# A tuned attention and two-layer MoE kernel: attention scores by 32-query chunks with their own 64 keys, instead of 128-row products with a mask

## Chip, cores and metric

The kernel runs on one core of a Trainium2 chip, in float32. The metric is the device time of one execution in microseconds, here the median of three runs: 516.09 us (515.79 to 516.44).

## What is computed

Attention over 2 batches x 8 heads x 768 positions with head dimension 64. Queries are taken in chunks of 32. A chunk sees 16 keys to its left, its own 32, 8 to its right, and 8 memory keys: 64 keys in all, fewer at the ends of a sequence.

```python
for c in range(S // 32):
    l_start, r_end = max(0, c * 32 - 16), min(S, c * 32 + 32 + 8)
    k_full = np.concatenate([mem_k, k[:, :, l_start:r_end]], axis=2)
    v_full = np.concatenate([mem_v, v[:, :, l_start:r_end]], axis=2)
    scores = scale * np.matmul(q_c, k_full.transpose(0, 1, 3, 2))
    a = np.exp(scores - np.max(scores, axis=-1, keepdims=True))
    a = a / (np.sum(a, axis=-1, keepdims=True) + 1e-09)
    out[:, :, chunk] = np.matmul(a, v_full)
```

The result (1536 tokens x 512) goes through a dense layer pair, `h = x @ w_in; g = h * sigmoid(1.702 h); y = g @ w_out` (512 to 2048 to 512), and then through a mixture of 8 experts with one expert per token (512 to 1024 to 512), of which each takes at most 384 tokens. All this behind the attention is the same in both kernels.

## The kernel before

**Tiles.** The 1536 tokens are 12 tiles (`NT`) of 128. In a tile there are two windows of 64 queries (`WINDOWS`, `HALF`) and four pairs of heads (`NP`): `NBL` = 8 blocks. A block is one pair of heads in one window. Its 128 rows are 64 queries of the first head and 64 of the second; its columns are `KEYS` = 96 keys: 64 + 16 + 8 and 8 memory keys. The two heads of a pair share one product over 128 contraction rows, 64 per head. For this `fill_block` copies the loaded queries (`queries`) into a block-diagonal arrangement in `tile_in`, whose other places `zero_blocks` cleared at the start. The copies are ScalarE's (two per tile), and for the first three tiles one of the two is VectorE's.

**Steps of a tile t.** `scores(t)` on TensorE: 8 products of 128 x 96 into two PSUM banks. `add_mask(t)` on VectorE adds the mask (keys outside a row's chunk get -1e30) and reduces the maximum over 96 keys. `less_max(t)` on GpSimd subtracts it, `exps(t)` on ScalarE takes the exponential, `inverse(t)` on VectorE sums and inverts, `normalise(t)` on GpSimd multiplies, `transposes(t)` on TensorE turns the 8 blocks, `copy_pT(t)` on ScalarE brings them to SBUF, `values(t)` on TensorE multiplies by the values (16 products of 64 columns, alternately for the upper and lower 64 partitions of the result), and `x_high(t)` (ScalarE) and `x_low(t)` (VectorE) split the result into two parts for the dense layer. A float32 product shows as two instructions in the profile.

**Order.** Every engine has a list written out by hand, and semaphores tie them. TensorE: `keep_warm` products on a constant, scores of tiles 0 to 2, more `keep_warm`, then for each t `transposes(t)`, `scores(t + 3)`, `values(t)`. With t = 8 the values move one place later; from t = 10 on `dense_hidden` takes the place of the scores. VectorE splits the first weight units (`split_lo`) in places 9 to 11, after ScalarE's `split_hi`.

**Loads.** All loads are issued by SyncE in program order: queries, keys and values of a tile as three transfers (256, 336 and 384 KB), a ring of three tiles (`NSLOT`), which waits for the copies, the scores and the values of the tile three before. The mask (288 KB) stands between the first and the second tile's loads. The weight units (512 KB) begin with t = 11 (`EARLY_FROM`).

Of the kernel before, what the change touches and what calls it, by code (L numbers as in the profile page):

```python
# [12 lines left out]
F32 = mybir.dt.float32  # L13
# [11 lines left out]
def build(nc, dims, attn_in, mask_in, w_units, w_gate_in, gate_rows_in, const_in, out):  # L25
# [11 lines left out]
    NBL = NP * WINDOWS  # L37
    BPG = NBL // 2
    GROUPS = [(g, g + BPG) for g in range(0, NBL, BPG)]
    NG = len(GROUPS)  # L40

    MAX_GROUPS = [GROUPS] + [[(0, NBL)]] * (B * S // P - 1)
    max_done = lambda t, g: sum(len(x) for x in MAX_GROUPS[:t]) + g + 1
    SCALE = 1.0 / D ** 0.5
    QK = NBL * P + NP * SPAN
    ATT = QK + WINDOWS * DM
    Q_IN = NBL * HALF
    NSLOT = 3
# [12 lines left out]
    EARLY_FROM = NT - 1  # L61
# [13 lines left out]
    WARM_FIRST, WARM_SECOND = 34, 35  # L75
# [15 lines left out]
    with ctx:  # L91
# [40 lines left out]
        queries = []  # L132
        for i in range(NSLOT):
            queries.append(at(f"queries{i}", [P, Q_IN], F32, o))
            o += Q_IN * 4
        prob, masked = [], []
        for i in range(2):
            prob.append(at(f"prob{i}", [P, NBL, KEYS + 1], F32, o))
            o += NBL * (KEYS + 1) * 4
        for i in range(2):  # L140
            masked.append(at(f"masked{i}", [P, NBL, KEYS], F32, o))
            o += NBL * KEYS * 4
        mask = at("mask", [P, 3, WINDOWS * KEYS], F32, o)
        o += 3 * WINDOWS * KEYS * 4
# [85 lines left out]
        score_bank, pT_bank, xT_bank = (bank[0:2], [bank[2], bank[5]]), bank[3:5], bank[6:8]  # L230
# [17 lines left out]
        s_block = [sem(f"s_block{i}") for i in range(2)]  # L248
        s_tiny = sem("s_tiny")
        s_v = [sem(f"s_v{i}") for i in range(NSLOT)]  # L250
        s_zero_q = sem("s_zero_q")
        s_mask_in = sem("s_mask_in")
# [6 lines left out]
        s_mask = sem("s_mask")  # L259
# [78 lines left out]
        def query_block(n, half, place):  # L338

            return tile_in[n][half * D:(half + 1) * D, 0:NBL * P].rearrange("p (x m) -> p x m", x=NBL)[
                :, :, place * HALF:(place + 1) * HALF]

        def fill_block(write, engine, t, half):
            n = t % NSLOT
            engine.wait_ge(s_q[n], 16 * (t // NSLOT + 1))
            if t >= NSLOT:
                engine.wait_ge(s_score, NG * (t - NSLOT + 1))
            there = queries[n][half * D:(half + 1) * D, :].rearrange("p (x m) -> p x m", x=NBL)  # L350
            write(query_block(n, half, half), there).then_inc(s_block[half], 1)
# [72 lines left out]
        def _(sp):  # L424
            def load_queries(t):
                n = t % NSLOT
                if t >= NSLOT:
                    for half in range(2):
                        sp.wait_ge(s_block[half], t - NSLOT + 1)
                sp.dma_start(queries[n][:, :], attn_in[t, :, 0:Q_IN]).then_inc(s_q[n], 16)  # L430

            def load_keys(t):
                n = t % NSLOT
                if t >= NSLOT:
                    sp.wait_ge(s_score, NG * (t - NSLOT + 1))
                sp.dma_start(tile_in[n][:, NBL * P:QK], attn_in[t, :, Q_IN:Q_IN + NP * SPAN]).then_inc(s_k[n], 16)

            def load_values(t):
                n = t % NSLOT
                if t >= NSLOT:  # L440
                    sp.wait_ge(s_pv, t - NSLOT + 1)
                there = attn_in[t, 0:KEYS, Q_IN + NP * SPAN:Q_IN + NP * SPAN + WINDOWS * DM]
                sp.dma_start(tile_in[n][0:KEYS, QK:ATT], there).then_inc(s_v[n], 16)
# [30 lines left out]
            for t in range(NSLOT, NT + NSLOT):  # L474
                if t < NT:
                    load_queries(t)
                    load_keys(t)
                if t == EARLY_FROM:
                    load_unit(unit)
                    unit += 1  # L480
                if t - NSLOT + 1 < NT:
                    load_values(t - NSLOT + 1)
                if t > EARLY_FROM:
                    load_unit(unit)
                    unit += 1
# [31 lines left out]
        def _(pool):  # L517
            pool.memset(empty_row[:, 0:DM + 1], 0.0).then_inc(s_empty, 1)
            pool.memset(empty_row[:, DM + 1:ROW], FAR).then_inc(s_empty, 1)
            pool.memset(ident[:, :], 0.0).then_inc(s_pool_c, 1)  # L520
            pool.memset(ones[:, :], 1.0).then_inc(s_pool_c, 1)
# [5 lines left out]

            def by_row(stats, x0, x1):
                return stats[:, x0:x1].rearrange("p (x a) -> p x a", a=1).to_broadcast([P, x1 - x0, KEYS])

            def less_max(t):
                for g, (x0, x1) in enumerate(GROUPS):
                    for n, some in enumerate(MAX_GROUPS[t]):
                        if some[0] == x0:
                            pool.wait_ge(s_max, max_done(t, n))
                    part = masked[t % 2][:, x0:x1, :]
# [1241 lines left out]
```

## Time and profile before

| what | value |
|---|---|
| median of 3 runs | 516.09 us |
| profiled execution | 516.33 us, span of the core 514.6 us |
| instructions | 8465 |
| busy share PE / PE weight load / DVE / ACT / POOL | 97 / 81 / 64 / 46 / 36% |
| TensorE clock granted (mean) | 0.995 of full speed |
| transfers | 77.17 MB, mean 150 GB/s |
| attention part | from the start to about 63 us, where the first output of the dense layer starts |

PE is TensorE's matmuls, PEld its weight loads, DVE VectorE, ACT ScalarE, POOL GpSimd, SPq the transfers issued from SyncE's queue. The busy shares are means over the whole span; the attention part is one eighth of it, and it has other limits than the rest. "L1271" is line 1271 of the kernel: L1271 are the scores, L1282 the transposes, L1298 the values, L1470 the warm-up products, L1306 to L1308 `dense_hidden`, L1350 to L1352 the dense outputs, L885 the mask add, L869 the maximum, L537 `less_max`, L543 `normalise`, L622 the exponential, L655 and L351 the query copies, L904 `x_low`, L430, L436 and L443 the issues of queries, keys and values, L373 `split_lo`.

### The profile page before, as it was taken

To read this page: it belongs to the slowest core of one execution; us is meant where nothing else is said; L and a number is where in the kernel's file an instruction comes from. 1 tells how busy PE (TensorE), PEld (TensorE's weight loads), DVE (VectorE), ACT (ScalarE), POOL (GpSimd) and SP (SyncE) were. 2 spreads that over 40 slices of the span, in tenths; PEclk is the share of its full clock that TensorE was granted. 3 is DMA by queue.
4 is the path that set the end of the run, shared out by engine and by line. 5 is a ranking of instruction groups with operands and counts; after the bars stand their busy time and mean duration, and the time that the engine had idled before them with its cause. 6 is when DMAs were issued, how large, how long until landed. Compare 5 with 4: busy or idle time off the path is not lost.

```text
span 514.6 us, 8465 instructions
## 1 busy us (share of the span) xinstructions
PE 497.4 (97%) x3013; PEld 418.7 (81%) x3013; DVE 327.1 (64%) x688; ACT 235.6 (46%) x416; POOL 186.3 (36%) x210
## 2 busy tenths in 40 slices
PE   7999999999999999999999999999999999999993
PEld 7898788888888887888888778888988888888882
DVE  7899765445237777323776877864577878638750
ACT  3899653343231122123122365523467768847620
POOL 3887400000000000300000017245337999999942
PEclk9999999999999999999999999999999999999998
DMA  8997799700020000100222236223796987956100
GB/s 260 257 265 235 279 357 332 249 3 0 2 82 2 0 1 0 58 26 36 88 82 83 82 101 227 82 75 107 234 343 212 351 329 263 356 211 230 39 28 33
DMA packets 28588, 77.17 MB, mean 150 GB/s; under 512 B 5487, under 2 KB 5487, under 8 KB 28272
## 3 DMA queue, kind: packets, MB, share of 16 engines
q1 hardware_dynamic: 24528, 70.07, 41.0%
q0 software_dynamic: 4000, 6.32, 3.4%
q8 instruction: 35, 0.57, 0.5%
q14 instruction: 25, 0.20, 0.1%
HBM read 63.21 MB, written 19.96 MB: 162 GB/s over the span
## 4 chain that ended last, share of the span: by engine, by line
PE 83%; DVE 6%; issue 4%; ACT 2%; POOL 1%; DMA 1%; DVEq 1%; SPq 0%; another core or an unknown queue 0%; ACTq 0%; POOLq 0%
PE bank L1306 9%; PE bank L1308 9%; PE bank L1307 9%; PE bank L1350 8%; PE bank L1351 8%; PE bank L1352 8%; PE bank L1319 7%; PE bank L1271 3%; PE bank L1577 3%; PE bank L1321 3%; PE bank L1579 2%; PE bank L1580 2%; PE bank L1581 2%; PE bank L1298 2%; PE bank L1282 2%
## 5 line engine op out<-in xcount | busy, mean ns | idle before, releaser
L557 POOL DMA_INDIRECT dispatched_rows<-rows,slot_idx x12 | 13.1, 1092 | 260.5 <-issue 157.6
L373 POOL TENSOR_TENSOR w_lo<-raw,w_hi 128x256 fp32r<-128x256 f32 x100 | 88.9, 923 | 9.5 <-ACT w_hi L357 9.5
L644 ACT ACTIVATE g<-bank 128x512 f32<-128x512 f32 x48 | 28.7, 598 | 126.9 <-PE bank L1308 126.8
L357 ACT ACTIVATE w_hi<-raw 128x1024 fp32r<-128x1024 f32 x80 | 82.0, 1050 | 0.1
L373 DVE TENSOR_TENSOR w_lo<-raw,w_hi 128x1024 fp32r<-128x1024 f32 (+1 forms) x61 | 72.0, 1190 | 8.8 <-ACT w_hi L357 7.7
L911 DVE SCALAR_TENSOR_TENSOR g<-g,bank 128x512 f32<-128x512 f32 x48 | 33.0, 687 | 69.1 <-ACT g L644 69.0
L1306 PE MATMUL bank<-x_hi,w_hi 128*128 128x512 f32 x192 | 76.1, 397 | 0.0
L1350 PE MATMUL bank<-w_hi,g_hi 128*128 128x512 f32 x192 | 76.0, 396 | 0.0
L1351 PE MATMUL bank<-w_lo,g_hi 128*128 128x512 f32 x192 | 75.8, 395 | 0.0
L1352 PE MATMUL bank<-w_hi,g_lo 128*128 128x512 f32 x192 | 75.8, 395 | 0.0
L1308 PE MATMUL bank<-x_hi,w_lo 128*128 128x512 f32 x192 | 75.6, 394 | 0.0
L1307 PE MATMUL bank<-x_lo,w_hi 128*128 128x512 f32 x192 | 75.4, 393 | 0.0
L1319 PE MATMUL bank<-e_in,w_hi 128*128 128x384 f32 (+1 forms) x224 | 61.4, 355 | 1.6 <-DVE gx_lo L1173 0.9
L916 DVE TENSOR_TENSOR g_lo<-g,g_hi 128x512 fp32r<-128x512 f32 x48 | 33.2, 693 | 32.8 <-ACT g_hi L651 32.1
L1321 PE MATMUL bank<-e_in,w_lo 128*128 128x192 f32 (+1 forms) x224 | 53.6, 239 | 0.0
L651 ACT ACTIVATE g_hi<-g 128x512 fp32r<-128x512 f32 x48 | 30.4, 632 | 41.9 <-DVE g L911 40.3
L1319 PEld LDWEIGHTS bank<-e_in,w_hi 128*128 128x128 f32 x224 | 42.0, 188 | 5.5 <-issue 2.0
L972 DVE SCALAR_TENSOR_TENSOR products<-rows,gate_rows 128x512 f32<-128x512 f32 x64 | 44.2, 690 | 1.7
L1350 PEld LDWEIGHTS bank<-w_hi,g_hi 128*128 128x128 f32 x192 | 36.1, 188 | 8.7 <-DVE g_lo L916 0.2
L1352 PEld LDWEIGHTS bank<-w_hi,g_lo 128*128 128x128 f32 x192 | 36.1, 188 | 8.6
L1308 PEld LDWEIGHTS bank<-x_hi,w_lo 128*128 128x128 f32 x192 | 36.0, 188 | 8.5
L1351 PEld LDWEIGHTS bank<-w_lo,g_hi 128*128 128x128 f32 x192 | 36.1, 188 | 8.5
(155 smaller groups left out, 904.1 us busy)
## 6 DMA issues: line engine op xcount, KB each, us to landing
raw<-expert_units SPq DMA_DIRECT2D x64, 512.0 KB, 6.6
raw<-dense_units SPq DMA_DIRECT2D x16, 512.0 KB, 6.5
dispatched_rows<-empty SPq DMA_DIRECT2D x26, 257.0 KB, 11.0
slot_rows<-dispatched_rows SPq DMA_DIRECT2D x26, 257.0 KB
tile_in<-attention_tiles SPq DMA_DIRECT2D x12, 384.0 KB, 4.5
tile_in<-attention_tiles SPq DMA_DIRECT2D x12, 336.0 KB, 5.6
queries<-attention_tiles SPq DMA_DIRECT2D x12, 256.0 KB, 4.8
gate_rows<-gate_rows SPq DMA_DIRECT2D x2, 1024.0 KB, 5.0
```

Of the source, the lines that this page charges most:

```text
L357: act.activation(w_hi[u % RING][:, :], raw[u % RING][:, :], ACT.Copy).then_inc(s_whi, 1)
L373: last = engine.tensor_tensor(w_lo[u % RING][:, part], raw[u % RING][:, part], w_hi[u % RING][:, part].bitcast(F32), ALU.subtract)
L916: dve.tensor_tensor(g_lo[i % 2][:, :], g32[i % 2][:, :], g_hi[i % 2][:, :].bitcast(F32), ALU.subtract).then_inc(s_glo, 1)
L972: link(dve.scalar_tensor_tensor(products[:, :], rows[:, j, 0:DM], 1.0, gate_rows[e // HALF_E][:, e % HALF_E, :], ALU.mult, ALU.mult, accum ...
L1306: pe.matmul(dst, hi[w_at], m_hi, start=first, stop=False)
L1307: pe.matmul(dst, hi[w_at], m_lo, start=False, stop=False)
L1308: return pe.matmul(dst, lo[w_at], m_hi, start=False, stop=last)
L1319: pe.matmul(both, w_hi[u % RING][:, c:c + P], parts[:, :, k, 0:cols], start=(k == 0), stop=False)
L1321: last = pe.matmul(h[:, 0:cols], w_lo[u % RING][:, c:c + P], x_high[:, k, 0:cols], start=False, stop=(k == KT - 1))
L1350: pe.matmul(banks[j][:, :], gh, hi[:, cols], start=(f == 0), stop=False)
L1351: pe.matmul(banks[j][:, :], gh, lo[:, cols], start=False, stop=False)
L1352: last = pe.matmul(banks[j][:, :], gl, hi[:, cols], start=False, stop=(f == nf - 1))
```

## The change

A block is now one chunk of 32 queries of four heads (`QUAD`): 8 blocks (`NBL`) of 4 x 32 = 128 rows, each with the 64 keys of its chunk (`OWN`). A block's scores are four products, one per head: 64 contraction rows (the head's half of the partitions), 32 query columns, 64 keys, each written to its own 32 partitions. The host places the memory keys so that a chunk's 64 keys are adjacent. Nothing has to be zero around the queries, so they are loaded straight into `tile_in`, and query copies, zeroing and the mask go. At the two ends of a sequence `edges` writes -1e30 over the keys that don't exist (4 of the 12 tiles). `less_max` is VectorE's and reads PSUM. The weights are still written 96 wide, with zeros where a chunk has no key (set once), so that transposes and values keep their sizes. The ring has four tiles, and the keys are issued by ScalarE. All eight blocks of a tile lie in one PSUM bank, and the transposed weights get four banks. Warm-up products: 32 and 24 instead of 34 and 35. The loads of gate weights and constants move to t = 7.

```diff
+    OWN = LEFT + CHUNK + RIGHT + M
+    QUAD = P // CHUNK
+    CPW = HALF // CHUNK
+    NBL = H // QUAD * (P // CHUNK)
+    BPG = NBL // WINDOWS
-    NSLOT = 3
+    PLACE = KEYS + 1
+    NSLOT = 4
+    LEAD = 3
-    WARM_FIRST, WARM_SECOND = 34, 35
+    WARM_FIRST, WARM_SECOND = 32, 24
...
+        def part_scores(t, x0, x1):
+            side = xT_bank[0] if PARTS[t][0][1] < NBL and x0 else score_bank[t % 2]
+            return side[:, x0 * OWN:x1 * OWN].rearrange("p (x k) -> p x k", k=OWN)
...
+        def load_keys(act, t):
+            n = t % NSLOT
+            if t >= NSLOT:
+                act.wait_ge(s_score, NG * (t - NSLOT + 1))
+            act.dma_start(tile_in[n][:, Q_IN:QK], attn_in[t, :, Q_IN:QK]).then_inc(s_k[n], 16)
...
# SyncE
-            for t in range(NSLOT):
+            for t in range(LEAD):
                 load_queries(t)
-                load_keys(t)
-                if t == 0:
-                    sp.dma_start(mask[:, :, :], mask_in).then_inc(s_mask_in, 16)
             load_values(0)
-            sp.dma_start(w_gate[:, :, :], w_gate_in).then_inc(s_const_in, 16)
-            sp.dma_start(const[:, :], const_in).then_inc(s_const_in, 16)
...
# GpSimd
+            pool.memset(ones[:, :], 1.0).then_inc(s_pool_c, 1)
             pool.memset(ident[:, :], 0.0).then_inc(s_pool_c, 1)
...
-            less_max(0)
             for t in range(NT):
-                if t + 1 < NT - 1:
-                    less_max(t + 1)
                 normalise(t)
...
# ScalarE
             for t in range(NSLOT):
-                blocks(t)
+                load_keys(act, t)
             for t in range(-2, NT + 1):
+                if 1 <= t <= NT and t != NT - 3:
+                    x_high(t - 1)
                 if 0 <= t < NT:
                     copy_pT(t)
-                if 1 <= t <= NT:
+                if t == NT - 3:
                     x_high(t - 1)
                 if t + 2 < NT:
                     exps(t + 2)
-                    if NSLOT <= t + 4 < NT:
-                        blocks(t + 4)
+                    if t + 2 + NSLOT < NT:
+                        load_keys(act, t + 2 + NSLOT)
...
# VectorE
+            def maximum(t, n):
+                x0, x1 = PARTS[t][n]
+                if n == 0:
+                    edges(t)
+                dve.wait_ge(s_score, NG * t + (NG if x1 == NBL else 1))
+                dve.tensor_reduce(neg_max[t % 2][:, x0:x1], part_scores(t, x0, x1), AX.X, ALU.max,
                                   negate=True).then_inc(s_max, 1)
+            def less_max(t, n):
+                x0, x1 = PARTS[t][n]
                 if t >= 2:
+                    dve.wait_ge(s_exp, parts_done(t - 2))
+                dve.wait_ge(s_max, parts_done(t, n))
+                dve.tensor_tensor(less[t % 2][:, x0:x1, :], part_scores(t, x0, x1), by_row(neg_max[t % 2], x0, x1),
+                                  ALU.add).then_inc(s_sub, 1)
...
+            for n in range(NG):
+                maximum(0, n)
+                less_max(0, n)
+            maximum(1, 0)
+            inverse(0)
+            less_max(1, 0)
+            maximum(2, 0)
+            less_max(2, 0)
+            for t in range(NT + 1):
+                if t + 1 < NT - 1:
                     inverse(t + 1)
                 if t == NT - 1:
                     gated(0)
+                if t >= 1:
                     x_low(t - 1)
+                if t + LEAD < NT:
+                    maximum(t + LEAD, 0)
+                    less_max(t + LEAD, 0)
                 if t == NT - 3:
+                    split_lo(dve, 0)
                     inverse(NT - 1)
...
# TensorE
+                for x0, x1 in GROUPS:
+                    dst = part_scores(t, x0, x1)
                     for x in range(x0, x1):
-                        q0, k0 = x * P, NBL * P + x // WINDOWS * SPAN + x % WINDOWS * (HALF + M)
-                        last = pe.matmul(score_bank[t % 2][g][:, (x - x0) * KEYS:(x - x0 + 1) * KEYS],
-                                         tile_in[n][:, q0:q0 + P], tile_in[n][:, k0:k0 + KEYS],
-                                         start=True, stop=True)
+                        w, g, c = x // BPG, x % BPG // CPW, x % CPW
+                        for j in range(QUAD):
+                            pair, side = (QUAD * g + j) // 2, slice(j % 2 * D, (j % 2 + 1) * D)
+                            q0 = pair * P + w * HALF + c * CHUNK
+                            k0 = Q_IN + pair * SPAN + w * (HALF + M) + c * CHUNK
+                            last = pe.matmul(dst[j * CHUNK:(j + 1) * CHUNK, x - x0, :], tile_in[n][side, q0:q0 + CHUNK],
+                                             tile_in[n][side, k0:k0 + OWN], start=True, stop=True)
...
-            pe.wait_ge(s_pool_c, 2)
+            pe.wait_ge(s_pool_c, 1)
             keep_warm(WARM_FIRST)
-            for t in range(NSLOT):
-                pe.wait_ge(s_zero_q, 2 * (t + 1))
+            for t in range(LEAD):
                 scores(t)
```

## Rows read from the trace of the kernel before

**Rows 1.** The page: busy time of each engine, share of the span, instructions.

```profile
PE 497.4 (97%) x3013; PEld 418.7 (81%) x3013; DVE 327.1 (64%) x688; ACT 235.6 (46%) x416; POOL 186.3 (36%) x210
```

**Rows 2.** Stretches: length, busy time of each engine, PE clock, DMA share, GB/s.

```profile
2.50:18.00 15.50, 13.40 (x140) 12.64 (x139) 11.76 (x25) 7.22 (x13) 7.61 (x10) 1.00 1.03 288
...
15.80:48.70 32.90, 32.90 (x468) 31.47 (x465) 29.49 (x50) 30.78 (x60) 27.40 (x35) 1.00 0.90 259
```

**Rows 3.** The chain of waits up to 70 us: start, duration, what.

```profile
2.18 4.85 DMA queries<-attention_tiles
...
19.00 1.01 PE bank L1282 x8
...
43.12 1.76 PE bank L1271 x16
44.88 1.08 PE bank L1298 x32
45.96 1.01 PE bank L1282 x8
46.97 1.77 PE bank L1271 x16
...
51.11 2.60 POOL prob L543 x2
...
54.40 0.23 PE bank L1306
...
63.29 0.43 PE bank L1350
```

**Rows 4.** The timeline of the attention part: start, duration, engine, line, operation.

```profile
1.24 0.42 SPq L436 DMA_DIRECT2D tile_in<-attention_tiles  x1
...
1.70 3.34 PE L1470 MATMUL bank<-ones 128*128 128x128 bf16 x34 [1.70 <-POOL ones L521]
...
4.88 1.98 PE L1271 MATMUL bank<-tile_in 128*128 128x96 f32 x16
...
7.95 2.00 PE L1271 MATMUL bank<-tile_in 128*128 128x96 f32 x16 [1.10 <-DMA tile_in<-attention_tiles]
...
12.25 2.12 PE L1470 MATMUL bank<-ones 128*128 128x128 bf16 x35
...
14.82 1.33 PE L1282 MATMUL bank<-ident,prob 128*96 128x128 f32 x8 [0.46 <-POOL prob L543]
...
51.76 1.25 DVE L373 TENSOR_TENSOR w_lo<-raw,w_hi 128x1024 fp32r<-128x1024 f32 x1
```

**Rows 5.** Values products (L1298) in flight, stretches of 10 ns; count in brackets.

```profile
25.54:25.55 0.01, 0.00 (x1) 1.00 0.78 205
25.55:25.56 0.01, 0.01 (x2) 1.00 0.00 0
...
25.66:25.67 0.01, 0.01 (x4) 1.00 1.31 410
...
25.72:25.73 0.01, 0.01 (x6) 1.00 2.33 614
```

**Rows 6.** Groups by shape from 0 to 62 us: busy us, mean ns, idle before.

```profile
L543 POOL TENSOR_TENSOR prob<-prob,prob_inv 128x384 f32<-128x384 f32 x24 | 20.3, 868 | 3.8 <-DVE prob_inv L899 3.1
...
L655 ACT ACTIVATE tile_in<-queries 64x512 f32<-64x512 f32 x21 | 13.1, 623 | 5.6 <-DMA queries<-attention_tiles 5.4
L885 DVE TENSOR_TENSOR masked<-bank,mask 128x384 f32<-128x384 f32 x24 | 12.8, 545 | 2.9 <-PE bank L1271 2.6 <-issue 0.3
...
L622 ACT ACTIVATE prob<-masked 128x384 f32<-128x384 f32 x24 | 11.6, 518 | 6.0 <-POOL masked L537 5.7
...
L869 DVE TENSOR_REDUCE neg_max<-masked 128x8 f32<-128x768 f32 x11 | 10.4, 948 | 0.3
L904 DVE TENSOR_TENSOR x_lo<-bank,x_hi 128x512 fp32r<-128x512 f32 x11 | 7.5, 682 | 0.4 <-ACT x_hi L636 0.4
...
L869 DVE TENSOR_REDUCE neg_max<-masked 128x4 f32<-128x384 f32 x2 | 1.1, 553 | 0.1
```

More of the change, by code:

```diff
@@ L131, in build @@
             o += ATT * 4
[L132 to L136, printed above, removed]
+        prob, less = [], []
         for i in range(2):
-            prob.append(at(f"prob{i}", [P, NBL, KEYS + 1], F32, o))
-            o += NBL * (KEYS + 1) * 4
+            prob.append(at(f"prob{i}", [P, NBL, PLACE], F32, o))
+            o += NBL * PLACE * 4
         for i in range(2):
[L141 to L144, printed above, removed]
+            less.append(at(f"less{i}", [P, NBL, OWN], F32, o))
+            o += NBL * OWN * 4
         probT = []
@@ L427, in load_queries @@
                 if t >= NSLOT:
[L428 to L434, printed above, removed]
                     sp.wait_ge(s_score, NG * (t - NSLOT + 1))
-                sp.dma_start(tile_in[n][:, NBL * P:QK], attn_in[t, :, Q_IN:Q_IN + NP * SPAN]).then_inc(s_k[n], 16)
+                sp.dma_start(tile_in[n][:, 0:Q_IN], attn_in[t, :, 0:Q_IN]).then_inc(s_q[n], 16)
             def load_values(t):
@@ L651, in g_high @@
                 act.activation(g_hi[i % 2][:, :], g32[i % 2][:, :], ACT.Copy).then_inc(s_ghi, 1)
-            def blocks(t):
-                for half in range(1 if t < NSLOT else 2):
-                    fill_block(lambda to, there: act.activation(to, there, ACT.Copy), act, t, half)
             for t in range(NSLOT):
-                blocks(t)
+                load_keys(act, t)
             for t in range(-2, NT + 1):
+                if 1 <= t <= NT and t != NT - 3:
+                    x_high(t - 1)
                 if 0 <= t < NT:
                     copy_pT(t)
-                if 1 <= t <= NT:
+                if t == NT - 3:
                     x_high(t - 1)
@@ new lines, in edges @@
+            def edges(t):
+                place = t % TPB
+                if place == 0:
+                    ends = part_scores(t, 0, BPG)[:, 0:BPG:CPW, 0:LEFT]
+                elif place == TPB - 1:
+                    ends = part_scores(t, NBL - BPG, NBL)[:, CPW - 1:BPG:CPW, OWN - RIGHT:OWN]
+                else:
+                    return
+                dve.wait_ge(s_score, NG * t + (1 if t == 0 else NG))
+                dve.memset(ends, -1e30).then_inc(s_edge, 1)
+                dve.wait_ge(s_edge, sum(x % TPB in (0, TPB - 1) for x in range(t + 1)))
@@ L1704 @@
     f32 = np.float32
+    memory_at = [w * (half + M) + 2 * CHUNK - M for w in range(2)]
+    key = np.arange(P + LEFT + RIGHT)
+    place_of = key + M * (key >= memory_at[0]) + M * (key >= memory_at[1] - M)
     attn = np.zeros((NT, P, q_in + H // 2 * span + 2 * DM), f32)
@@ L1716 @@
         for wide, own, memory in ((kw, k, mem_k), (vw, v, mem_v)):
-            wide[:, M + lo - s0 + LEFT:M + hi - s0 + LEFT] = own[b, :, lo:hi]
-            wide[:, 0:M] = memory[b]
-            wide[:, span - M:] = memory[b]
+            wide[:, place_of[lo - s0 + LEFT:hi - s0 + LEFT]] = own[b, :, lo:hi]
+            for at in memory_at:
+                wide[:, at:at + M] = memory[b]
         attn[t, :, q_in:q_in + H // 2 * span] = kw.reshape(H // 2, 2, span, D).transpose(1, 3, 0, 2).reshape(P, -1)
@@ L1723 @@
             attn[t, 0:keys, at:at + DM] = vw[:, w * (half + M):w * (half + M) + keys].transpose(1, 0, 2).reshape(keys, DM)
-    mask = np.full((P, 3, 2, keys), -1e30, f32)
-    for r in range(P):
-        u0 = r % half // CHUNK * CHUNK
-        for w in range(2):
-            at = M * (1 - w) + u0
-            mask[r, :, w, at:at + LEFT + CHUNK + RIGHT] = 0.0
-    mask[:, 0, 0, M:M + LEFT] = -1e30
-    mask[:, 2, 1, keys - M - RIGHT:keys - M] = -1e30
-    mask[:, :, 0, 0:M] = 0.0
-    mask[:, :, 1, keys - M:] = 0.0
-    mask = mask.reshape(P, 3, 2 * keys)
     def in_units(w):
@@ L1764 @@
     nc = bacc.Bacc("TRN2", target_bir_lowering=False, num_devices=1)
-    arrays = {"attention_tiles": attn, "masks": mask, "dense_units": dense, "expert_units": experts,
+    arrays = {"attention_tiles": attn, "dense_units": dense, "expert_units": experts,
               "gate_weights": gate_w, "gate_rows": gate_rows, "constants": const}
```

192 lines of the change are left out of this document (73 added, 119 removed).

## The prediction

> **What bounds the kernel now.** I read the page's engine line first: the span is 514.6 us and PE is busy for 97% of it [rows 1]. That says only that PE seldom waits, so I asked next for the stretches. Between 15.8 and 48.7 us, nearly the whole attention part that the change touches, PE is busy all the time, ACT 94%, DVE 90%, POOL 83%, and the DMA engines move 259 GB/s at a share of 0.90 [rows 2]. Four engines and the DMA are within 17% of the same limit, so a part taken from DVE, ACT or POOL gives nothing by itself. The chain of waits decides: from 19.0 to 48.7 us it holds PE alone, in a pattern of three groups per tile, transposes 1.01, scores 1.76, values 1.08 [rows 3]. The sum, 3.85 us, is the pitch; the pattern stands eight times. At the ends other engines enter the chain. At the start the second tile's queries land at 7.03 us [rows 3], and the first transposes start at 14.82 [rows 4]. At the end POOL's normalisation takes 2.60 us of the chain, the first dense product starts at 54.40 and the first dense output at 63.29 [rows 3]. After that nothing is touched, so I count until there: what the change saves at 63.29 it saves in the whole.
>
> **Scores on PE, the deciding term.** Now a tile has 8 products of 128 x 96, two instructions each: 16 in 1.76 us, 110 ns apiece [rows 3]. After the change it has 8 x 4 = 32 products, with half the contraction (64), 32 columns of stationary operand and 64 moving columns: 64 instructions. No such shape is in the trace. Nearest is the values product: also 64 moving columns, stationary 64 wide, its results going alternately to the two halves of the partitions. Its starts come two at a time: the count of those in flight goes 1, 2, then 4 at 25.66 and 6 at 25.72 [rows 5], and 32 take 1.08 us [rows 3]. So after a first gap of 110 ns a pair costs about 59 ns, an instruction 29.5 ns. Three readings fit: fp32 operands stream at about half speed (53 ns for 64 columns at 2.4 GHz), two column groups at a time; or the two passes run one after the other at full speed (26.7 ns each); or the 64-column load is the limit. The transposes, 8 in 1.01 us with 128 moving columns and only 96 loaded, against 110 ns for 128 loaded in the scores [rows 3], speak for a streaming limit. Under the first two readings 64 moving columns cost what they cost in values: 64 x 29.5 = 1.89 us. The shape of the array changes once more per tile (the transposes and the scores now use the same one, later they don't), for which I take the 0.11 us of the first gap in values. Sum 2.00 us, so 0.24 us more per tile than now, and a pitch of 1.01 + 2.00 + 1.08 = 4.09 us. Bounds: below, the third reading, a load half as wide, 32 pairs of 29 to 32 ns, 1.0 + 0.11 = 1.1 us; above, no overlap at all, 64 x 59 = 3.8 + 0.11 = 3.9 us. I take 2.00, the row with the same moving width.
>
> The Trainium skill (TensorE: Matmul & The Clock Gate, "Wait — 56ns, not 53.3ns?") gives a floor of about 25 ns between starts of matmuls; the pairs that start within 10 ns [rows 5] don't obey it, but as a mean rate it would make 64 x 25 = 1.6 us, between my value and the lower bound.
>
> **DVE, ACT, POOL.** DVE loses the mask add (2 x 545 ns) and gets the subtraction of the maximum from POOL. That is 512 elements now, as long as x_lo from PSUM, 682 ns. The reductions shrink from 768 to 512 elements: between 553 (384) and 948 (768) that is 685 ns, twice [rows 6]. Per tile 0.68 + 0.68 + 0.69 + 0.20 (the reciprocal) + 0.68 = 2.9 us where it is 3.9. ACT loses the query copies (2 x 623), its exponential becomes one of about 0.6 us (now 2 x 518 [rows 6]), and it gets one issue of keys, at most the 0.42 us that it takes on SyncE's queue [rows 4]; behind that issue stand the next tile's copies, which have the slack: 2.7 us of 4.09. POOL keeps the normalisation with 256 instead of 384 elements, about 0.57 instead of 0.87 each [rows 6], 1.1 us. All this lies beside PE's 4.09 and costs nothing; if PE's groups came to 1.1 us, DMA and not these would be next.
>
> **DMA.** The bytes per tile stay: 262 + 344 + 393 KB = 1.00 MB. Gone are the 0.29 MB of masks, and the gate weights and constants go behind. While the queue is saturated, from 2.5 to 18 us, it moves 288 GB/s [rows 2]: 3.47 us per tile, under 4.09, so the transfers are hidden, but nothing below 3.47 can be had.
>
> **The start, step by step.** Warm-up products start at 1.70 now [rows 4] because `ones` is the fourth memset; it becomes the first, and they end near 4.3. The first queries and keys (0.61 MB) land at about 4.8, so the first scores run 4.8 to 6.8; the copies and zeroing are no longer before them, but the start (4.88 now [rows 4]) stays. For the second tile 1.21 MB must have come. Now 1.16 MB are ahead of the queries' landing at 7.03 [rows 3] (mask included), so scores(1) runs from 7.2 (now 7.95) to 9.2, scores(2) to 11.2 with its data there by 9.3 (0.61 MB at 288 GB/s later), 24 warm-up products at 56 ns (35 in 2.12, the last's 0.22 taken off [rows 4]) to 12.6. On DVE max(1) waits for scores(1) until 9.3, inverse(0) follows it, and the first half's normalisation is done near 11.2, so it is not late. Transposes(0) start at 12.6 instead of 14.82: 2.2 us gained.
>
> **The middle.** Now it is 4.1 us from transposes(0) to (1), which stand in the chain at 19.00, and then 3.85 for each tile, to 45.96 for tile 8 [rows 3]. After: 12.6 + 8 x 4.09 = 45.3, last scores done at 45.3 + 3.0 = 48.3 instead of 48.74 [rows 3]. Of the 2.2 us, 0.4 are left.
>
> **The end.** Now 54.40 - 48.74 = 5.66 us pass before the first dense product, with 2.0 of transposes and 2.16 of values in it; the rest is waiting, mostly for POOL, whose two normalisations of tile 10 stand in the chain with 2.60 us [rows 3]. After: transposes(9) to 49.3, values(8) and (9) to 51.4; DVE does max and subtraction of tile 11 to 49.8, inverse(10) to 50.7, POOL to 51.9, transposes(10) to 52.4. Late next is DVE's split of the first weight unit: behind x_lo(8), which waits for values(8) and ACT until 51.0, it runs from 51.7 for 1.25 us [rows 4] and ends at 52.95. There the dense product starts, 1.45 us earlier. Then 2.75 (hidden) + 1.08 + 1.0 + 2.75 + 1.08 = 8.66 us against 8.89: first output at 61.6 instead of 63.29. Sum: 1.7 us gained.
>
> The profiled execution took 516.33 us, 1.73 above its span, and the median of the runs is 516.09, 0.24 below it. Taken off the median: 514.4 us.
>
> **Rivals.** (A) Products of 32 columns overlap better, as in the third reading. For: four column groups where values have two. Against: the transposes. With groups of 1.1 us the pitch would be 3.2, but DMA holds it at 3.47, and scores(11) waits for 10.8 MB, that is until about 3.0 + 37.5 = 40.5; it would end at 41.7, 7.0 us earlier, and with the shorter end 508.6 us. At the 1.6 us rate, pitch 3.8: 9 x 0.29 and 2 x 0.29 before transposes(0), 3.2 us better than forecast, 511.2.
> (B) Slower: products in the upper and the lower half of the contraction rows alternate and write one PSUM bank, and they don't overlap or they pay a change each. There are 11 score groups on the path (2 ahead of transposes(0), 9 in the middle), so it turns to a loss when a group exceeds 2.00 + 1.7/11 = 2.15 us, 33 ns an instruction. At 40 ns it is 2.7 us and 522; with no overlap 3.9 us, 1.9 x 11 = 21 more, 535. For: the trace shows pairs only in one row group. Against: they go to different partitions, as the pairs of values do. The skill states (TensorEngine Tiling (Array Packing), "Gotcha 1: PSUM Pressure") that different row tiles cannot access the same PSUM bank at once; taken literally that is the 535 case. No row here shows it either way.
> (C) The change does less than it says at the ends (the transposes stay late because the first loads from two queues finish together, the split is later still): the pitch's 0.24 x 9 stays and 1 of the gains goes: 515.5 to 517.
>
> **Chances.** Forecast 0.46 (own range 513.2 to 515.8), A 0.27 (508.5 to 512.5), B 0.18 (half of it under 520), C 0.09. The range 508.5 to 518.5 leaves out most of B. A difference under 0.2% (1.03 us) can't be told from none: faster holds A and three quarters of the forecast, 0.61; same the rest of it and part of C and B, 0.17; slower 0.22.
>
> **What would show it.** The score group's time in the chain: 2.0 right, 1.1 to 1.7 A, above 2.15 B. Transposes(0) at 12.6; pitch 4.09 with PE alone in the chain; DVE, ACT and POOL each idle over a quarter of the stretch; first dense product at 53.0, held by the split. If DMA appears among PE's waits in the middle, the term for PE was too high.

## The result, and the profile after

The changed kernel takes 522.84 us (median of 11 runs, 518.12 to 524.39), the kernel before in the same comparison 516.20. The ratio of their runs is 1.0109, 95% interval 1.0083 to 1.0136: 1.1% slower. I had forecast 514.4, in a range of 508.5 to 518.5. The runs are also more scattered: 6.3 us from lowest to highest, before 1.8 us.

The page of the changed kernel, its engine line, the clock granted to TensorE in 40 slices, and the queue that carries instructions:

```profile
PE 494.5 (95%) x3576; PEld 412.7 (79%) x3576; DVE 312.9 (60%) x678; ACT 219.8 (42%) x384; POOL 161.1 (31%) x186
...
PEclk9789899999999999999999999999999999999997
...
q8 instruction: 39, 0.64, 0.5%
```

PE has 563 matmuls more than in [rows 1] and yet less busy time. In the attention part the clock is now below full speed again and again.

Three stretches of the changed kernel, with the columns of [rows 2]:

```profile
12.30:15.80 3.50, 1.66 (x15) 1.49 (x16) 1.10 (x2) 0.00 (x0) 0.00 (x0) 0.50 1.03 301
15.80:48.70 32.90, 28.86 (x836) 25.20 (x835) 21.10 (x41) 17.21 (x31) 9.55 (x16) 0.90 0.93 255
48.70:63.30 14.60, 11.30 (x184) 9.20 (x180) 8.90 (x16) 7.91 (x13) 4.57 (x6) 0.88 0.72 242
```

The relief on DVE, ACT and POOL came as forecast: 64, 52 and 29% of the middle stretch, where it was 90, 94 and 83% [rows 2]. But PE, busy all the time before, now idles 4 us of these 32.9, and none of the other engines is near its limit.

The chain of waits of the changed kernel (start, duration, what), the answer to [rows 3]. L1264 are the scores, L1274 the transposes, L1289 the values, L1462 the warm-up products, L1298 the first dense product, L1342 the first dense output:

```profile
9.70 1.09 PE bank L1264 x62
10.79 3.34 issue
14.14 0.42 PE bank L1264 x2
14.55 2.67 PE bank L1462 x24
17.23 1.71 PE bank L1274 x8
...
22.17 1.03 PE bank L1264 x64
23.20 1.08 PE bank L1289 x32
24.28 1.01 PE bank L1274 x8
...
28.41 0.62 PE bank L1264 x33
29.02 0.62 issue
...
32.38 0.91 PE bank L1264 x55
33.29 2.30 issue
35.59 0.32 PE bank L1264 x9
35.91 1.78 PE bank L1289 x32
37.69 1.87 PE bank L1274 x8
...
45.26 1.13 issue
...
50.21 0.39 PE bank L1264 x17
50.60 2.65 issue
...
60.35 0.47 PE bank L1298
...
69.27 0.43 PE bank L1342
```

Two things stand in it. A score group takes 1.03 us, not 1.76 as before and not the 2.00 that I forecast; three groups together take 3.12 us. And five times PE stops for 0.6 to 3.3 us, 10.04 us in all, with "issue" as the cause: no semaphore, no transfer of data. It stops in the middle of a group, in scores(2) between instruction 62 and 63 of 64, where no wait stands in the code. In the same stretch, 9 to 56 us, PE has no such stop in the kernel before (the one "issue" piece over 0.1 us of that chain, 0.44 us at 48.80, is VectorE's). Behind a long stop groups run at half speed: values in 1.78 instead of 1.08, transposes in 1.87 instead of 1.01, with the granted clock at 0.56 of full speed between 35.6 and 39.5 us (mostly its lower level, 1.2 GHz). The first dense output starts at 69.27 where it was 63.29 [rows 3]: 5.98 us later. The spans differ by 5.7 us (520.3 and 514.6), so all of the loss is made ahead of that point.

The places of the stops count. Between one stop and the next lie 126 pairs of weight load and matmul, 252 instructions: from 29.64 to 33.29 it is 31 + 32 + 8 + 55 = 126, from 46.39 to 50.60 it is 5 + 64 + 32 + 8 + 17 = 126. Between stops further apart there are 252 pairs (35.59 to 45.26) and 379 (14.14 to 29.02), twice and, within one, three times 126. The few waits between them make up the rest. Numbered with its waits, as the trace records them, the instruction at which PE goes on is number 449, 1217, 1474, 1986 and 2242: the distances are 768, 257, 512 and 256, within one a multiple of 256 each time. The instruction queue moves 0.64 MB in 39 packets, 16.4 KB each, that is 64 bytes for each of 256 instructions. A packet of this queue shows up shortly before each end of a stop. One stretch of 0.25 us, 33.00 to 33.25, shows it; 28.4% of 16 engines' time is 1.14 us, the time that this one packet took:

```profile
q8 instruction: 1, 0.02, 28.4%
```

| packet starts | has landed | PE goes on | from landing to PE |
|---|---|---|---|
| 11.51 | 12.70 | 14.14 | 1.44 |
| 27.18 | 28.41 | 29.64 | 1.23 |
| 33.08 | 34.22 | 35.59 | 1.37 |
| 43.88 | 44.76 | 46.39 | 1.63 |
| 50.55 | 51.69 | 53.25 | 1.56 |

So what PE waits for has the time of an instruction packet. It is the landing that counts: in e10 below one packet took 2.31 instead of about 1.2 us (from 41.58 to 43.89), and PE went on 1.47 us behind its end. The kernel before has such packets too, at 15.7, 23.8, 31.1 and 42.2 us, but 126 pairs last 8.7 us there (56 pairs per tile of 3.85 us), here 3.8 us (104 pairs per 3.12 us).

### The profile page after: what moved, and what is told of

It reads as the page before. It is cut to its first block, busy times and chain, and to the rows that moved or that the text cites. A ratio compares the mean times of both kernels' runs of the same rounds, so it can differ in the third digit from the quotient of the medians.

```text
span 520.3 us, 9477 instructions
## 1 busy us (share of the span) xinstructions
PE 494.5 (95%) x3576; PEld 412.7 (79%) x3576; DVE 312.9 (60%) x678; ACT 219.8 (42%) x384; POOL 161.1 (31%) x186
## 3 DMA queue, kind: packets, MB, share of 16 engines
q0 software_dynamic: 4000, 6.32, 3.4%
## 4 chain that ended last, share of the span: by engine, by line
PE 87%; issue 4%; DVE 3%; ACT 2%; DMA 2%; ACTq 0%; POOL 0%; POOLq 0%; DVEq 0%
PE bank L1298 9%; PE bank L1300 9%; PE bank L1299 9%; PE bank L1342 8%; PE bank L1343 8%; PE bank L1344 8%; PE bank L1311 7%; PE bank L1568 3%; PE bank L1313 3%; PE bank L1274 3%; PE bank L1570 2%; PE bank L1572 2%; PE bank L1571 2%; PE bank L1289 2%; PE bank L1264 2%
## 5 line engine op out<-in xcount | busy, mean ns | idle before, releaser
L1298 PE MATMUL bank<-x_hi,w_hi 128*128 128x512 f32 x192 | 76.1, 396 | 0.7 <-DVE w_lo L383 0.7
L1342 PE MATMUL bank<-w_hi,g_hi 128*128 128x512 f32 x192 | 76.0, 396 | 0.0
L1311 PE MATMUL bank<-e_in,w_hi 128*128 128x384 f32 (+1 forms) x224 | 61.6, 356 | 1.2 <-DVE gx_lo L1162 0.8
L1298 PEld LDWEIGHTS bank<-x_hi,w_hi 128*128 128x128 f32 x192 | 36.0, 188 | 9.1 <-issue 0.9
L1342 PEld LDWEIGHTS bank<-w_hi,g_hi 128*128 128x128 f32 x192 | 36.1, 188 | 8.7 <-DVE g_lo L906 0.2
```

The costliest lines, as they stand in the source:

```text
L1298: pe.matmul(dst, hi[w_at], m_hi, start=first, stop=False)
L1311: pe.matmul(both, w_hi[u % RING][:, c:c + P], parts[:, :, k, 0:cols], start=(k == 0), stop=False)
L1342: pe.matmul(banks[j][:, :], gh, hi[:, cols], start=(f == 0), stop=False)
```

## The experiments

Theory F: PE outruns the supply of its own instructions, which come over the same busy DMA engines. The stall sums below are PE's idle pieces of over 0.1 us without a releaser, from 9 to 56 us of one profiled execution. That execution is one of the runs and not always a typical one: those of e6 (517.10 us), e9 (514.40), e10 (518.59) and e12 (516.44) stand at the low end of theirs, those of e11 (518.36) and e14 (520.30) at the top.

| kernel | median us | ratio to before (95%) | stalls us (count) |
|---|---|---|---|
| before | 516.20 | | 0 |
| after | 522.84 | 1.0109 (1.0083 to 1.0136) | 10.0 (5) |
| e1 keys by SyncE | 524.73 | 1.0163 (1.0144 to 1.0181) | 12.4 (5) |
| e10 split transfers | 520.85 | 1.0089 (1.0072 to 1.0105) | 7.1 (4) |
| e5 wide warm-up | 521.65 | 1.0100 (1.0081 to 1.0120) | 9.6 (5) |
| e6 and ring of three | 519.63 | 1.0065 (1.0041 to 1.0090) | 6.5 (6) |
| e9 and split transfers | 517.58 | 1.0016 (0.9995 to 1.0038) | 5.7 (7) |
| e13 and split units | 516.78 | 1.0005 (0.9984 to 1.0026) | 7.3 (8) |
| e14 = e9, 3 warm-up products | 518.04 | 1.0019 (1.0004 to 1.0035) | 9.4 (8) |
| e11 finer, none, three | 517.12 | 1.0002 (0.9990 to 1.0014) | 4.7 (5) |
| e12 finer, none, four | 518.59 | 1.0037 (1.0023 to 1.0050) | 6.1 (8) |

The medians come from different comparisons, so the ratios are what to compare. e2, e3, e4 and e7 leave out or change a part of the computation and have one execution each (525.82, 524.79, 523.31 and 530.04 us); they are read by their chains in the attention part, not by these times.

**e1: the keys back on SyncE's queue.**

```diff
             for t in range(LEAD):
                 load_queries(t)
+                load_keys(sp, t)
```

> The changed kernel with one part undone: the keys are issued by SyncE again, right behind each tile's queries; all else stays. Theory F (PE starves for its own instructions: they come in pieces of 16 KB over the same DMA engines, 252 weight loads and matmuls apiece; the score products use up a piece in under 4 us, and behind saturated data queues a piece takes 3.7 to 6.7 us): a second data queue may lengthen the wait of a piece, so the stalls without a releaser (10.0 us in sum in the chain of the changed kernel) should fall somewhat, to 5 to 9 us, and stay at multiples of 126 pairs; time 515 to 522. Rival Q (the keys over ScalarE's queue are what costs): the stalls go, time 509 to 512. Rival R (the alternation of the two row halves in one PSUM bank stalls PE): nothing changes, 10 us of stalls at the same places, 521 to 523.

Measured 524.73 us, above my 515 to 522, and 12.4 us of stalls where I expected 5 to 9. The two longest are 4.12 us in scores(2) and 3.94 us in scores(7); the one in scores(6) shrinks to 0.07, and one of 0.90 us appears 28 instructions into values(0), which is 126 pairs behind the first. ScalarE's queue isn't the cause; rival Q falls, and so does my side remark that a second queue lengthens the wait. That the places stay multiples of 126 apart suits F; R, too, had expected the old ones to stay.

**e2: most of the later values left unloaded.**

```diff
+                end = ATT if t < NSLOT else QK + P
-                sp.dma_start(tile_in[n][0:KEYS, QK:ATT], attn_in[t, 0:KEYS, QK:ATT]).then_inc(s_v[n], 16)
+                sp.dma_start(tile_in[n][0:KEYS, QK:end], attn_in[t, 0:KEYS, QK:end]).then_inc(s_v[n], 16)
```

> The changed kernel, but from the fifth tile on only 128 of the 1024 value columns are loaded (that part of the computation is changed, with stale values for the rest): 8 x 0.34 MB fewer, so the DMA engines are no longer saturated, and PE's instructions are the same. Theory F: the wait from the request of an instruction piece to its landing falls to about 3 us, the stalls behind 27 us (6.7 us in sum: 0.62, 2.30, 1.13, 2.65) go or fall under 1 us, the pitch is 3.12 us throughout and the first dense product starts at about 52 instead of 60.3 us. Rival R: the stalls stay, as PE's work is the same. Rival Q: they stay in part, since ScalarE's queue still carries the keys.

Its whole time can't be compared: wrong values behind the attention probably send other tokens to other experts, which was not looked at. Behind 25 us PE stops for 0.48, 0.27, 0.72 and 1.07 us, 2.5 in sum where the changed kernel has 6.7 (a piece of 0.55 us in the same chain is VectorE's, one of 0.14 us follows POOL). The first dense product starts at 53.16 (forecast about 52) instead of 60.35, the first dense output at 61.95 instead of 69.27. Fewer bytes, same PE instructions, under half the stalls: R can't explain that. But they don't fall under 1 us in sum as I expected: even with the DMA engines at 0.68 of their time (28 to 46 us; 0.97 in the changed kernel from 27 to 50) some pieces come too late.

**e3: all products from one row half.**

```diff
-                            pair, side = (QUAD * g + j) // 2, slice(j % 2 * D, (j % 2 + 1) * D)
+                            pair, side = (QUAD * g + j) // 2, slice(0, D)
```

> The changed kernel with all score products taken from the lower 64 partitions (the heads of the upper half are computed from the wrong rows), so the row half never alternates; number, shapes and order of instructions are the same. It asks why a score group takes 1.03 us (16 ns an instruction) where I had forecast 1.89. If the overlap comes from four column groups alone, the group stays at 1.03. If the two row halves are what lets products run side by side, it grows to about 1.9 us. Rival R (alternating halves in one bank cause the stalls): the stalls without releaser vanish. Theory F: with a group still 1.03 they stay; with 1.9 they shrink because a piece lasts longer.

The chain: a group of 64 in 1.03 us (22.56 to 23.58), stops of 2.21, 0.89, 1.47, 0.58 and 4.01 us at the same five places. Their sum is 9.2 us (10.0 in the changed kernel). The alternation of the row halves neither helps nor hurts; R falls. My 535 case came from the rule that different row tiles cannot access the same PSUM bank at once (the Trainium skill, TensorEngine Tiling (Array Packing), "Gotcha 1: PSUM Pressure"), read literally. It has no support in these shapes: the changed kernel alternates the row halves in one bank at 16 ns an instruction.

**e4: 32 instead of 64 moving columns.**

```diff
+                            m = OWN if t < 3 else CHUNK
...
+                                             tile_in[n][side, k0:k0 + m], start=True, stop=True)
```

> The changed kernel with score products of 32 instead of 64 moving columns from the fourth tile on (the other 32 keys' scores are left stale): 64 instructions of half the streaming. If the group of 1.03 us is bound by streaming (64 columns), it falls towards 0.6 us; if by the 32-column load or by issue (16 ns per instruction), it stays at 1.0. The stalls stay by theory F, and grow a little if the group gets shorter.

The timeline of PE in this kernel (start, duration; the duration counts the last product to its end):

```profile
43.06 0.76 PE L1265 MATMUL bank<-tile_in 64*32 64x32 f32 x64
43.75 1.15 PE L1290 MATMUL bank<-probT,tile_in 96*64 96x64 f32 x32
```

From start to start the group takes 0.69 instead of 1.03 us. So the group of 1.03 us is bound by the moving columns and not by the load, which was the same. It doesn't fall to half, so a part of it doesn't go with the columns. Stalls: 13.9 us, longest 3.90: with shorter groups they grow, as F says.

**e7: half of the score products.**

```diff
-                        for j in range(QUAD):
+                        for j in range(QUAD if t < 3 else QUAD // 2):
```

> The changed kernel with only the first two heads' products of each block from the fourth tile on (the other rows keep stale scores): 32 instead of 64 score instructions, 72 pairs per tile instead of 104, all loads as before. PE alone would need 1.01 + 0.55 + 1.08 = 2.64 us per tile. Theory F: a piece of 126 pairs then lasts over 4.6 us, and 6 if the pitch is held at 3.47 by the transfers, so the stalls without releaser behind 20 us fall under 1.5 us in all (6.7 in the changed kernel), though the transfers are as dense. The chain shows DMA instead, at a pitch of 3.3 to 3.6 us. A rival in which dense transfers alone stall PE keeps 5 us or more of stalls.

The chain of this kernel:

```profile
24.79 1.01 PE bank L1274 x8
25.80 1.01 PE bank L1264 x32
26.81 1.08 PE bank L1289 x32
```

I expected 0.55 us for the 32 instructions and measured 1.01. That tells the width of the overlap: with results for two column groups (here: the 32 partitions of the result that one head's product writes) an instruction costs 31.6 ns, with four 16 ns. Within one column group it is 63 to 64 ns either way. The kernel has 72 pairs per 3.1 us, a piece lasts 5.4 us, and between 20 and 46 us one stall is left, 0.60 us (in the changed kernel 0.62 + 2.30 + 1.13), with the DMA engines as busy (0.97). So with fewer instructions per microsecond the supply mostly suffices. But one stall of 3.03 us at 46.45 remains, 3.6 us in all behind 20 us and not under 1.5 as I expected. Its packet starts at 46.89, 6.5 us after PE passed the boundary before it (40.4 us by the count). In this run DMA holds the chain once, from 35.4 to 45.7 us, for one transfer; PE itself waits 0.25 us for it.

**e5: the same warm-up with fewer instructions.**

```diff
-    WARM_FIRST, WARM_SECOND = 32, 24
+    WARM_FIRST, WARM_SECOND = 8, 6
...
-                    pe.matmul(bank[7][:, 0:P], ones[:, :], ones[:, :], start=True, stop=True)
+                    pe.matmul(bank[7][:, :].rearrange("p (a q) -> p a q", a=4), ones[:, :], wide, start=True, stop=True)
```

> The changed kernel with 8 and 6 warm-up products of 512 columns in place of 32 and 24 of 128: the same streaming, 42 pairs of weight load and matmul fewer on PE before the transposes. Theory F says the places of the stalls are places in the instruction stream (pair 222 from the first warm-up product, then every 126th): all move 42 pairs on. The first, now after 62 of the 64 instructions of scores(2), moves into scores(3) after 8 instructions, behind transposes(0), so scores(2) isn't cut and transposes(0) start near 11.5 to 12.5 instead of 17.2 us; scores(3) waits there until about 14. The next places: 30 instructions into scores(4), 52 into scores(5), 10 into values(3), the end of values(4). 2.5 to 5 us faster than the changed kernel: 518 to 520. Rival D (a wait for data, the third tile's keys, which the profile doesn't name): the stall stays in scores(2) after 62 instructions, and the time stays.

The chain of this kernel:

```profile
9.25 1.10 PE bank L1264 x64
10.34 1.40 PE bank L1463 x6
11.74 0.87 PE bank L1274 x8
12.62 0.24 PE bank L1264 x7
12.86 1.06 issue
...
17.03 0.57 PE bank L1264 x30
17.61 3.84 issue
...
34.60 1.08 PE bank L1289 x32
35.68 0.95 issue
36.63 1.03 PE bank L1274 x8
...
40.78 0.35 PE bank L1264 x14
41.13 3.18 issue
```

This is the plainest evidence. The stops lie where the count of instructions puts them: at the start of scores(3) (7, forecast 8), 30 instructions into scores(4), behind values(4). By the numbering with waits PE goes on at 449, 705, 1474, 1730 and 2242: the same numbers as in the changed kernel, or multiples of 256 from them, though other products stand there now. Data or PSUM know nothing of this count; D falls. Transposes(0) start at 11.74 instead of 17.23. Yet the time is only 1.2 us shorter, above my 518 to 520, and by the intervals it can't be told from the changed kernel's. The early gain of 5.5 us was given back, because the second stop became 3.84 us long, with half clock after it. Where PE is earlier, it meets the next piece earlier.

**e6, e9: what stands ahead of a piece.** e6 has a ring of three tiles; e9 also loads the values in four and the keys in two transfers.

```diff
-    NSLOT = 4
+    NSLOT = 3
...
+                for a in range(QK, ATT, DM // 2):
+                    sp.dma_start(tile_in[n][0:KEYS, a:a + DM // 2], attn_in[t, 0:KEYS, a:a + DM // 2]).then_inc(s_v[n], 16)
```

> As e5, with a ring of three tiles instead of four, so that fewer transfers are queued ahead when an instruction piece is asked for. Theory F with a queueing part: the stalls behind 25 us get shorter, 1 to 3 us in all less than in e5, 515.5 to 518.5. If the time of a piece is not set by how many transfers stand ahead, it equals e5 within 1 us; where PE now waits for data itself, it is slower.

> As e6 (wide warm-up products, three tiles in the ring), with the values loaded as two... four transfers of a quarter and the keys as two halves by columns: the same bytes in shorter pieces per engine. If an instruction piece waits for whole data packets ahead of it in the DMA engines, its wait falls and the stalls of e6 (6.4 us in sum behind the start) shrink by 1 to 3 us: 516.5 to 518.5. If it waits for the bytes, or the many small packets cost more, nothing or a loss: 519.5 to 523.

e6: 519.63 (forecast 515.5 to 518.5), e9: 517.58 us (forecast 516.5 to 518.5). The intervals of e5 and e6 overlap at the edge, so the gain from the shorter ring, 2 us by the medians, is likely and not certain here. Those of e6 and e9 don't overlap: the same bytes in shorter packets take 2 us off. The longest stall is 3.84 us in e5, 2.29 in e6, 1.38 in e9, and the granted clock between 15.8 and 48.7 us, 0.90 after the change, is 1.00 in e9. In e6 the places forecast for scores(5) (52 instructions) and values(3) (10) both appear. e9's profiled execution is its shortest (514.4 us), so its stalls are rather the lower end; e6's is near its own.

**e10: the split alone.** The same edit of the loads on the changed kernel.

> The changed kernel with one edit: the values come as four transfers (a quarter of the columns each) and the keys as two; the same bytes over the same queues, the same PE instructions at the same places. Theory F with data packets ahead of an instruction piece: the stalls (10.0 us in sum) stay at pairs 222, 600, 726 and so on, and get shorter, to 4 to 7 us in all; time 517.5 to 520.5 against the changed kernel's 522.8. If only the wide warm-up and the shorter ring had helped in e9, this one is at 522 to 523.

520.85 us (forecast 517.5 to 520.5): stops of 2.71, 2.29, 1.69 and 0.45 us at four of the old five places, and one of under 0.1. Its interval (1.0072 to 1.0105) overlaps that of the change at its edge, so the 2 us are likely and not certain.

**e8: only instructions added, to the kernel before.** Six `wait_ge` for a count long reached ahead of every transpose, value product and (from the fourth tile on) score product; in the trace they are three instructions.

> The kernel BEFORE, its computation untouched, with 3 empty instructions (waits for a count reached long ago) ahead of each transpose, score and value product on PE: 96 more instructions per tile, as many as the change adds (48 weight loads and 48 matmuls). Nothing of the change is in it: no small products, keys on SyncE's queue, mask and copies in place. It tests whether the number of PE instructions is enough. Theory F: a piece of 256 instructions now lasts 4.7 us of the 3.85 us tiles where it lasted 8.8, so gaps without a releaser of 0.5 to 3 us appear between 15 and 55 us, whole pieces apart, 2 to 8 us in sum, wherever the landing of a piece is late, and the time rises to 518 to 525. Rival R or D (the small products or their data): PE stays without gaps, 516 to 517. If an empty instruction itself takes long (over 40 ns), the groups of PE stretch evenly instead; then only gaps of over 0.3 us count.

Inconclusive, and I had mispriced it. The kernel took 603.8 us. One of its stretches (columns of [rows 2]):

```profile
41.30:53.00 11.70, 11.67 (x56) 8.90 (x56) 3.74 (x6) 3.67 (x7) 3.22 (x4) 0.50 0.28 85
```

The granted clock is 0.50 in it, and stays there at least until 110 us. So its groups can't be held against those of full speed, and a score group of 3.70 us, little more than twice 1.76, doesn't tell what a wait costs. A value group takes 5.02 us with 48 wait instructions, 105 ns each, and where PE has nothing else to do, from 17.41 to 17.73 us, such instructions start 106 ns apart in the trace. That is their price: 96 of them are 10 us, and a tile lasts 11.8 us. The instruction packets come 13.3 to 14.4 us apart (15.67, 28.95, 42.65 and 57.03), further than before the change. It doesn't test the supply.

**e11, e12: finer still, and without the second warm-up.** Queries and the first eight weight units in two transfers; ring of three and of four.

> As e9, and further: queries in two transfers and the first eight weight units in two, no warm-up products behind the third scores (6 wide ones in e9). Theory F: transposes(0) start about 1.4 us earlier (11.2 us), the stalls behind 25 us shrink from 4.4 to 2 to 4 us in sum: 514 to 516.5, at or under the kernel before. If the clock falls for want of warm-up products, the first tiles run at half speed and it gains nothing.

> As e11 with the change's ring of four tiles. If what an instruction piece waits for is the length of the packets, it equals e11 within 1 us; if it is the amount queued, it is 1 to 3 us slower than e11, 516 to 519.

517.12 us (forecast 514 to 516.5) and 518.59 us (forecast 516 to 519). The ring of three is better by 1.5 us, intervals apart: the amount queued counts too, not the packets' length alone. Without products behind the third scores, transposes(0) in e11 start at 11.89 but take 1.88 us, and values(1) take 1.90: the lower clock takes the gain. From 29 to 46 us the chain of e11 runs over SyncE's issues, six in a tile, mostly 0.43 us each and once in a tile 1.06 to 2.24 us, and PE waits for data twice (1.62 us at 39.75, 1.22 us at 44.57). So split further, the issues on SyncE hold PE up; why the long ones are long was not looked at.

**e13, e14: units split, half the warm-up.**

> As e9 (wide warm-up products 8 and 6, three tiles in the ring, values in four and keys in two transfers), with the first eight weight units in two transfers each. If the weight units' long packets hold the instruction pieces between 40 and 50 us, the two stalls there (0.47 and 1.38 us in e9) halve, 0.5 to 1 us gained: 516 to 517.2. If not, it equals e9 (517.6) within 0.5 us.

> As e9 with 3 instead of 6 wide warm-up products behind the third scores: 0.7 us less streaming. If the clock stays at its upper level, transposes(0) start 0.7 us earlier and the time falls by 0.3 to 0.7 us. If the thinner start brings the lower level, as with none in e11 (transposes(0) in 1.88 instead of 1.01 us and half speed for a tile or two), it loses 0.5 to 2 us against e9.

516.78 and 518.04 us (e9: 517.58). Neither can be told from e9 by the intervals. e13's time lies in the range of my first case (516 to 517.2), but not by its mechanism, as its stalls show. In e14 transposes(0) start at 11.33, 1.3 us earlier than in e9, but a stop of 1.96 us follows and values(0) take 1.85 at the lower clock. In e13 the late stalls (0.90 and 2.49 us, in e9 0.47 and 1.38) didn't halve in the execution profiled, which speaks against the weight units' packets as what holds them. No version beats the kernel before; e9, e11 and e13 can't be told from it.

## Why the prediction was wrong

- **The step that turned the sign: "a pitch of 1.01 + 2.00 + 1.08 = 4.09" with PE busy throughout.** I put the supply of PE's instructions at nothing, without a reason, and it stood in no rival. I counted 64 instructions for 16 as time on the array, never as bytes: a tile's 208 weight loads and matmuls instead of 112, in 3.12 instead of 3.85 us, are a 16 KB packet every 3.8 instead of 8.7 us. The runs show 10.0 us of stops, and the half clock behind them: transposes(0), values(4), transposes(5) and the second warm-up are 0.70 + 0.70 + 0.86 + 1.33 = 3.6 us too long, and behind the last stop the rest of scores(11) and transposes(9) another 1.6. The first dense output is 7.7 us later than forecast (69.27 for 61.6): 4.6 at the start, 1.8 in the middle, 1.0 before the first dense product, 0.3 behind it. The profile of the kernel before had the signs: 35 packets, 0.57 MB in all, on the instruction queue, DMA at 0.90 of its time [rows 2]. The Trainium skill has the rule that I didn't weigh (Runtime: NRT & Kernel Launch, "Instruction fetch mechanics"): instructions come in blocks of 16 KiB, 256 of them, over a DMA queue. The block size agrees with 16.4 KB here. It calls the cost of a boundary mostly hidden; with PE at 30 ns per pair or less under full DMA engines the runs show up to 4.1 us (e1).
- **The term that was mis-sized: "Scores on PE, the deciding term".** I took 29.5 ns an instruction, 2.00 us a group; it is 16 ns and 1.03 us. My first reading of the pairs in [rows 5] had fp32 streaming as the limit, which e4 bears out, but I carried over "two column groups at a time" where the change has four. e7 shows the two sides: 31.6 ns with two groups, 16 with four. The lower bound (1.1 us) was near it, for another reason than the one I gave; the rate of 1.6 us a group didn't hold either. This error alone would have made the kernel faster than forecast, towards rival A; that is argued, as no run has the short groups without the stops. (A's own sum is off as well: a middle 6.6 us shorter than forecast and the same end give 507.8 us, not 508.6.)
- **The pitch came near by luck.** From transposes(0) to transposes(8) it is 32.0 us, 4.0 a tile where I had 4.09: 3.12 us of work plus stops and half clock, not a group of 2.00.
- **"DVE, ACT, POOL": right.** The profile after has 691 (maximum), 689 (subtraction), 685 (sum), 651 (x_lo) and 631 ns (exponential), forecast about 685, 682, 685, 682 and 600; POOL has 659 for 570 ns, 16% more, which cost nothing.
- **"DMA": "nothing below 3.47 can be had" fails for a few tiles.** The pitch was 3.12 us for the tiles between stops, from a ring filled ahead; PE's stops then gave the transfers time. Whether 3.47 binds in the long run stays unsettled.
- **"The start": right until the first stop.** Scores(0) start at 4.79 (forecast 4.8), scores(1) at 6.32 (forecast 7.2, 0.9 too late), scores(2) got their data at 9.7 (forecast 9.3). Then the stop of 3.34 us and the warm-up at the lower clock, 1.33 us too long: transposes(0) at 17.23 instead of 12.6, the largest single miss, 4.6 us.
- **"The end": right in kind.** The first dense product waits for VectorE's split of the first unit, which ends at 60.2 us; 5.6 us from the last scores to it, forecast 4.65.
- **Rival B gave the right sign by a wrong mechanism.** e3 refutes it.

What stays open: when PE asks for a piece. Counting the boundaries by 256 instructions, each packet of the changed kernel starts 1.2 to 4.2 us after PE has passed a boundary and is needed at the next, 3.8 us later at full pace. That fits a request made at the boundary, but no run isolates it. Open, too, is how the wait divides between the number of queued transfers (e6, e12) and their length (e9), and why the clock falls behind some stops and not behind others.

## What to carry to other kernels

Count instructions per microsecond on PE as a load on the DMA engines. With these nearly full, 256 instructions in 3.8 us gave five stops at eight boundaries (changed kernel), 256 in 5.4 us gave two stops at five boundaries behind 20 us (e7), and 256 in 8.7 us none (before). When a split of products packs them this densely, look for "issue" gaps in the middle of a group, whole multiples of one count apart. A group that becomes cheaper on the array shortens the very time that hid the fetch: e4, with still shorter groups, has 13.9 us of stops. Shorter transfers and a shallower ring relieve it, 1.5 to 2 us each here; wide warm-up products only moved the stops (e5).

## What was not expected of the hardware

- Four column groups run side by side: 16 ns an fp32 instruction of 64 columns, against 31.6 ns with two and 64 ns within one (e7, changed kernel).
- From the landing of an instruction packet to PE's next instruction it is 1.2 to 1.6 us in all five stops (2.5 to 2.7 us from the packet's start).
- A wait instruction whose count is long reached costs 105 ns on PE where nothing hides it (e8), over six times a small score instruction.
- Behind the stop at 33.29 us (2.30 us) the granted clock was 0.56 from 35.6 to 39.5 us; behind the one at 45.26 (1.13 us) the groups kept the lengths that they have at full speed.
